# 56 expert blocks of two sizes in place of 55 of one size, with another order of products in the small ones

## What is computed

```python
X = np.fft.fft(np.fft.fft(x, axis=1), axis=2).real
# experts: D = 256, F = 1024, E = 8
expert_idx = np.argmax(logits, axis=1)
for e in range(E):
    mask = expert_idx == e
    h = np.maximum(x[mask] @ w1[e], 0.0)
    out[mask] = gate_w[mask, None] * (h @ w2[e])
# channel mix of 24 tiles of 512 tokens: x_k, x_r from x and the token before
k = np.maximum(xk @ w_k, 0.0)
v = k * k @ w_v
r = 1.0 / (1.0 + np.exp(-(xr @ w_r)))
return r * v
```

## Time and profile before

| | |
|---|---|
| median of three runs | 1440.82 us |
| profiled execution, its own time | 1442.9 us |
| its span, first to last instruction | 1440.9 us |
| busy: matmuls (PE) / VectorE (DVE) / ScalarE (ACT) / GpSimd (POOL) | 97% / 76% / 61% / 17% |
| mean granted TensorE clock | 0.989 |
| expert stage: products of the first and second layer, busy | 324.7 and 328.7 us |

### The profile page before, as it was taken

How to read it: one execution, slowest core, us unless ns; L and a number is a source line. 1 busy time by engine, 2 the same in 40 slices (tenths; PEclk the granted TensorE clock), 3 DMA queues, 4 the chain that set the end, 5 groups by cost and what they waited for, 6 DMA issues and landing times.

```text
span 1440.9 us, 27303 instructions
## 1 busy us (share of the span) xinstructions
PE 1403.9 (97%) x9048; PEld 1282.2 (89%) x9048; DVE 1088.1 (76%) x1815; ACT 872.3 (61%) x1687; POOL 250.8 (17%) x225
## 2 busy tenths in 40 slices
PE   8999989998999999999999969999999999999998
PEld 7988879998999999999999958888888888888886
DVE  4788887876776777777677657878788887878784
ACT  2665576665766666666666546656565666656563
POOL 2154537551331111111111100000000000000000
PEclk8999999999999999999999989999999999999999
DMA  8334378899667677777766322212131313131201
GB/s 243 84 102 130 119 240 277 270 292 322 221 212 226 218 219 218 228 240 235 227 216 219 132 45 40 49 32 55 29 58 29 58 29 58 29 58 29 57 17 29
DMA packets 208343, 201.49 MB, mean 140 GB/s; under 512 B 189641, under 2 KB 191543, under 8 KB 199672
## 3 DMA queue, kind: packets, MB, share of 16 engines
q1 hardware_dynamic: 197336, 175.18, 42.9%
q0 software_dynamic: 9888, 25.28, 5.3%
q10 hardware_dynamic: 1056, 0.26, 0.1%
HBM read 160.44 MB, written 42.06 MB: 141 GB/s over the span
## 4 chain that ended last, share of the span: by engine, by line
PE 91%; DVE 3%; DMA 2%; SPq 1%; ACT 1%; issue 1%; POOL 0%; ACTq 0%; POOLq 0%; DVEq 0%
PE ps L626 82%; PE ps L654 3%; PE ps L694 3%; PE ps L679 1%; DMA we_raw<-w_e 1%; PE ps L680 1%; DMA rows<-xr,pos 1%; DVE zu L1171 1%; DVE zv L1171 1%; SPq L455 0%; DVE we L1146 0%; SPq L540 0%; DMA xm<-moe 0%; ACT we L817 0%; PE ps L631 0%
## 5 line engine op out<-in xcount | busy, mean ns | idle before, releaser
L626 PE MATMUL ps<-x_split,w_split 128*128 128x512 f32 x1440 | 332.3, 391 | 11.3 <-DVE x_split L1293 11.3
L626 PE MATMUL ps<-we,ht 128*128 128x256 f32 x2640 | 328.7, 283 | 4.8 <-DVE ht L1229 4.8
L626 PEld LDWEIGHTS ps<-x_split,w_split 128*128 128x128 f32 x1440 | 271.6, 189 | 68.1 <-issue 11.5
L626 PE MATMUL ps<-xgt,we 128*128 128x256 f32 x2640 | 324.7, 282 | 4.3 <-DVE we L1146 4.3
L626 PEld LDWEIGHTS ps<-we,ht 128*128 128x128 f32 x2640 | 322.1, 189 | 6.4 <-DVE ht L1229 6.1
L626 PEld LDWEIGHTS ps<-xgt,we 128*128 128x128 f32 x2640 | 319.4, 190 | 4.7 <-issue 4.7
L1146 DVE TENSOR_TENSOR we<-we_raw,we 128x1024 fp32r<-128x1024 f32 x220 | 263.9, 1221 | 22.6 <-ACT we L817 22.1
L626 PE MATMUL ps<-k_split,w_split 128*128 128x512 f32 x1152 | 265.0, 389 | 0.0
L626 PEld LDWEIGHTS ps<-k_split,w_split 128*128 128x128 f32 x1152 | 216.2, 188 | 44.9
L1229 DVE SCALAR_TENSOR_TENSOR ht<-ps,ht 128x512 fp32r<-128x512 f32 x220 | 146.1, 684 | 144.4 <-ACT ht L878 144.2
L817 ACT CAST we<-we_raw 128x1024 fp32r<-128x1024 f32 x220 | 225.1, 1048 | 8.3 <-DMA we_raw<-w_e 8.3
(11 more groups left out here) (131 smaller groups left out, 1085.4 us busy)
## 6 DMA issues: line engine op xcount, KB each, us to landing
we_raw<-w_e SPq DMA_DIRECT2D x55, 2048.0 KB, 8.3
xg<-rows SPq DMA_DIRECT2D x220, 64.0 KB
out<-yc SPq DMA_DIRECT2D x96, 128.0 KB, 2.7
xm<-moe SPq DMA_DIRECT2D x94, 128.0 KB, 2.8
xin<-x SPq DMA_DIRECT2D x15, 768.0 KB, 6.5
rows<-tailc SPq DMA_DIRECT2D x9, 258.0 KB, 9.2
moe<-yo,meta POOLq DMA_INDIRECT x110
rows<-xr,pos POOLq DMA_INDIRECT x96, 2.7
```

The costliest lines, as they stand in the source:

```text
L626: ins = mm(o, a(i), b_(k), start=first_ and n == 0, stop=last_ and n == 2)
```

## The change

The constants now give 47 blocks of 256 tokens and 9 of 128 (`NS`), together `NB` = 56. `blocks` takes the place of `pairs`: 18 large blocks unrolled, then nine passes of a hardware loop with four blocks each (`MIX`), of which the fourth is small, then two large ones. The semaphore counts are rewritten with `at_`, `ahead`, `turn` and `scattered_ahead` for the two sizes; loads, transposes and scatters of a small block handle 128 tokens.

A small block's first layer uses each high weight once, with the high and the low part of the rows side by side as 256 columns, and each low weight with the 128 high columns. So a PSUM bank holds, for each of two slices, a half k=0 (high x high plus low x high) and a half k=1 (high x low). ScalarE copies the second half out (`half_b`), VectorE adds the first (`sum_one`), ScalarE makes the high part by a ReLU (`hidden_one`), VectorE the remainder (`low_one`). The second layer has one token half and 24 products.

The lists get a third kind of step. Large blocks of tier 2 are counted by rounding down, an expert with an odd half block gets one small block, and the small blocks left over are the halves of further large ones (`tier_odd`, `tier_odd2`, `tier_odd3`, `tier_spare`, `tier_spare2`, at the ends of VectorE's steps 7 to 11; `tier_a` to `tier_e` move to steps 4 to 6). The last of them adds the third count to `d_tier`, and `load_tails` waits for three. The diff, cut to its core:

```diff
-NB = B * S // BT + E - 1
-TIERS = ((0, 17), (17, 38))
+NS = 9
+NP = (B * S // P + E - 1 - NS) // 2
+NB = NP + NS
+MIX = 4
+TIERS = ((0, 17), (17, NP - 17))
+LIST = TIERS[1][1] + (NS + 1) // 2
...
+        def one(i):
+
+            return i[1] == MIX - 1 if isinstance(i, tuple) else LEAD <= i < LEAD + MIX * NS and (i - LEAD) % MIX == MIX - 1
+
+        def tokens(i):
+
+            return P if one(i) else BT
...
+        def blocks(eng, step):
+
+            for i in range(LEAD):
                 step(i, i % 2)
-            m = (n - lead - 1) // 2
-            with eng.Fori(0, m) as t:
-                for s in range(2):
-                    step(t * 2 + (lead + s), (lead + s) % 2)
-            for i in range(lead + 2 * m, n):
+            with eng.Fori(0, NS) as t:
+                for r in range(MIX):
+                    step((t, r), r % 2)
+            for i in range(LEAD + MIX * NS, NB):
                 step(i, i % 2)
 
...
             def load_meta(i, s):
 
-                r = sp.value_load(row_of[0:1, bass.ds(i, 1)], min_val=0, max_val=E * CAPR)
+                n = tokens(i)
+                r = sp.value_load(row_of[0:1, bass.ds(i, 1)], min_val=0, max_val=XROWS - n)
                 if i >= LEAD + 2:
-                    sp.wait_ge(scattered[s], i // 2 * (16 * HB))
-                sp.dma_start(meta_of(i, s)[:], rows[bass.ds(r, BT), D:ROW].rearrange("(j p) c -> p j c", j=HB)
+                    sp.wait_ge(scattered[s], scattered_ahead(i, s))
+                sp.dma_start(meta_of(i, s)[:, 0:n // P], rows[bass.ds(r, n), D:ROW].rearrange("(j p) c -> p j c", p=P)
                              ).then_inc(meta_in[s], 16)
...
             def load_tails():
 
-                sp.wait_ge(d_tier, 2)
+                sp.wait_ge(d_tier, 3)
...
+                n = tokens(i)
                 w1_ = [we[s][:, k, 0:DC * F].rearrange("p (c f) -> p c f", c=DC) for k in range(2)]
                 for f in range(FC):
                     if f % 2 == 0:
-                        wait(pe, m_hl, (i - 1) * (FC // 2) + (f // 2 + 1))
+                        wait(pe, m_hl, (at_(i) - 1) * (FC // 2) + (f // 2 + 1))
+                    if one(i):
+                        o = ps[:, f // 2, f % 2 * BT:(f % 2 + 1) * BT].rearrange("p (k t) -> p k t", k=2)
+                        for c in range(DC):
+                            hi, lo = [w1_[a][:, c, f * P:(f + 1) * P] for a in range(2)]
+                            if c == DC - 1:
+                                mm(o[:, 0, :], lo, xgt[:, 0, c, 0:P], start=False, stop=False)
+                            last = mm(o, hi, xgt[:, :, c, 0:P], start=(c == 0), stop=(c == DC - 1))
+                            if c < DC - 1:
+                                mm(o[:, 0, :], lo, xgt[:, 0, c, 0:P], start=False, stop=False)
+                        if f % 2:
+                            last.then_inc(m_up, 1)
+                        continue
                     for c in range(DC):
-                        last = mm3(ps[:, f // 2, (f % 2) * BT:(f % 2 + 1) * BT],
+                        last = mm3(ps[:, f // 2, (f % 2) * n:(f % 2 + 1) * n],
                                    lambda a: w1_[a][:, c, f * P:(f + 1) * P],
-                                   lambda k: xgt[:, k, c, :], c == 0, c == DC - 1)
+                                   lambda k: xgt[:, k, c, 0:n], c == 0, c == DC - 1)
...
+            def half_b(i, n):
+                act.wait_ge(m_up, at_(i) * (FC // 2) + (n + 1))
+                copy(h_b[n % 2], ps[:, n, :].rearrange("p (f k t) -> p f k t", f=2, k=2)[:, :, 1, :]).then_inc(m_hb, 1)
+
+            def hidden_one(i, n):
+                act.wait_ge(m_hs, i[0] * (FC // 2) + (n + 1))
+                if n == 0:
+                    wait(act, m_down, ahead(i, HB, 1))
+                nc.scalar.activation(ht[:, 0, 2 * n:2 * n + 2, 0:P], h_s[n % 3], ACT.Relu).then_inc(m_hh, 1)
+
+            def m_one(i, s):
+                half_b(i, 0)
+                w_high_part(after(i), 1 - s, 0)
+                half_b(i, 1)
+                hidden_one(i, 0)
+                half_b(i, 2)
+                hidden_one(i, 1)
+                w_high_part(after(i), 1 - s, 1)
+                half_b(i, 3)
+                hidden_one(i, 2)
+                hidden_one(i, 3)
+                rows_a(after(i))
+                w_high_part(after(i), 1 - s, 2)
+                w_high_part(after(i), 1 - s, 3)
+                result(i, s, 0)
...
+            def tier_spare2():
+
+                total_odd = sums[1][:, 4 + E:5 + E]
+                t_link(v.tensor_scalar(late1[:], iota[0:1, 0:NS], total_odd, None, ALU.is_ge))
+                for out_, h, none, dst in ((where1, 0, E * CAPR, row_of), (who1, 1, E - 1, expert_of)):
+                    t_link(v.scalar_tensor_tensor(out_[:], late1[:], -float(none), out_[:], ALU.mult, ALU.add))
+                    t_link(v.tensor_tensor(out_[:], out_[:], got1[:, h, :], ALU.add))
+                    end = copy(dst[:, mixed].rearrange("o (t r) -> o t r", r=MIX)[:, :, MIX - 1], out_[:])
+                end.then_inc(d_tier, 1)
...
+            def sum_one(i, n):
+                dve.wait_ge(m_hb, i[0] * (FC // 2) + (n + 1))
+                if n == 3:
+                    dve.wait_ge(m_hl, at_(i) * (FC // 2) + 1)
+                v.tensor_tensor(h_s[n % 3], ps[:, n, :].rearrange("p (f k t) -> p f k t", f=2, k=2)[:, :, 0, :], h_b[n % 2],
+                                ALU.add).then_inc(m_hs, 1)
+
+            def low_one(i, n):
+                h = [ht[:, k, 2 * n:2 * n + 2, 0:P] for k in range(2)]
+                dve.wait_ge(m_hh, at_(i) * (FC // 2) + (n + 1))
+                v.scalar_tensor_tensor(h[1], h_s[n % 3], 0.0, h[0].bitcast(F32), ALU.max, ALU.subtract).then_inc(m_hl, 1)
+
+            def m_one(i, s):
+                rows_t(after(i), 1 - s)
+                sum_one(i, 0)
+                sum_one(i, 1)
+                low_one(i, 0)
+                sum_one(i, 2)
+                low_one(i, 1)
+                w_low_part(after(i), 1 - s, 0)
+                sum_one(i, 3)
+                low_one(i, 2)
+                low_one(i, 3)
+                rows_v(after(i), 1 - s)
+                for q in range(1, WP):
+                    w_low_part(after(i), 1 - s, q)
...
                     if i == 4:
                         tier_a(True)
+                        tier_a2(True)
                     if i == 5:
-                        tier_a2(True)
+                        tier_b(True)
+                        tier_c(True)
                     if i == 6:
-                        tier_b(True)
+                        tier_d(True)
+                        tier_e(True)
                     if i == 7:
-                        tier_c(True)
+                        tier_odd()
                     if i == 8:
-                        tier_d(True)
+                        tier_odd2()
                     if i == 9:
-                        tier_e(True)
-
-            pairs(dve, LEAD, NB, m_step)
+                        tier_odd3()
+                    if i == 10:
+                        tier_spare()
+                    if i == 11:
+                        tier_spare2()
+
+            blocks(dve, m_step)
```

More of the change, by code:

```diff
@@ L256, in fft_moe_channel_mix @@
         assert at[0] <= cw_at
+        at[0] = 0
+        h_b = [part(f"h_b{n}", [2, P]) for n in range(2)]
+        h_s = [part(f"h_s{n}", [2, P]) for n in range(3)]
+        assert at[0] <= early
         at[0] = cw_at
@@ L742, in m_step @@
                 down(i, s)
-            pairs(pe, LEAD, NB, m_step)
+            blocks(pe, m_step)
             for n in range(2):
                 pe.wait_ge(s_split[n], len(C_SPLIT_AT))
-            pe.wait_ge(m_y, NB * HB)
+            pe.wait_ge(m_y, ahead(NB, HB, 1))
             def c_step(t, s):
@@ L890, in m_step @@
             def m_step(i, s):
+                if one(i):
+                    m_one(i, s)
+                    return
                 more = not isinstance(i, int) or i + 1 < NB
-                hidden_a(i, 0)
+                for n in range(FC // 2):
+                    hidden_a(i, n)
+                    if more and n < 2:
+                        w_high_part(after(i), 1 - s, n)
                 if more:
-                    w_high_part(i + 1, 1 - s, 0)
-                hidden_a(i, 1)
-                if more:
-                    w_high_part(i + 1, 1 - s, 1)
-                hidden_a(i, 2)
-                hidden_a(i, 3)
-                if more:
-                    rows_a(i + 1)
-                    w_high_part(i + 1, 1 - s, 2)
-                    w_high_part(i + 1, 1 - s, 3)
+                    rows_a(after(i))
+                    w_high_part(after(i), 1 - s, 2)
+                    w_high_part(after(i), 1 - s, 3)
                 if isinstance(i, int) and i in C_SPLIT_AT:
@@ L915, in m_step @@
                     exponential(B - 1)
-                for j in range(HB):
+                for j in range(tokens(i) // P):
                     result(i, s, j)
```

(45 more changed lines are left out.)

172 lines of the change are left out of this document (113 added, 59 removed).

## The result

The changed kernel takes 1464.66 us (median of 4 runs, 1462.04 to 1468.42) beside 1440.62 us for the kernel before (4 runs, 1439.21 to 1442.13): 1.0169 times as long, 95% interval 1.0144 to 1.0193. Forecast were 1470.6 us and a range of 1452 to 1486. The profiled execution of after took 1462.04 us (span 1460.1); that of before 1442.9 (span 1440.9). So the two traces differ by 19.2 us and the medians by 24.0: after's profiled execution is the shortest of its runs, and before's is longer than its other runs.

A forecast was written before the change was run, and what follows sets the result against it. TensorE, busy 97% of the span, was taken to bound the kernel. Loop +8.3 and lead +21.5 make 29.8 us: 1442.9 + 29.8 = 1472.7, from the 2.1 lower median 1470.6 us; range 1452 to 1486.

The forecast's parts named there:

- both mechanisms: Lead: tail stores on SP wait for the odd list, +21.5 us; loop: late weight loads hold up small blocks' followers, +8.3 us.
- Two large blocks in the loop: In the loop over experts, a large block takes 11.45 us, two take 22.9 us.
- The small block: In the loop, a small block takes 9.3 us, not the 6.5 us of TensorE alone.
- the timetable: Small block, engine by engine: TensorE done at 8.26 us, then waiting for VectorE's weight part 1 until 9.3.
- Its follower: Block behind a small one: its cast waits 2.1 us for weights landing at 13.6; the pair takes 22.55 us.
- The loop's sum: Loop after the lead: 9 x (22.55 + 22.9) + 22.9 = 432.0 us against 423.7, +8.3 us.
- The lead: First blocks: tails on SP wait for the odd list, delaying rows and weights queued behind; +21.5 us, bounds 14 to 24.
- The total: Whole kernel: 8.3 + 21.5 = 29.8 us more, 1470.6 us as median.
- The loads don't bind: Rival, loop: loads land sooner or ScalarE's order absorbs them; pair 20.75 us, loop -8 us, total 1454; chance 0.12.
- Faster: Rival, loop: small blocks cost only TensorE's 6.5 us; loop -33 us, total 1429 with the lead's loss; chance 0.05.
- The clock falls as well: Rival, loop: waits lower TensorE's clock, 1.5 us a fall; one each round +13 us, 1484, two 1497; chance 0.15.
- The cover of the lead: Rival, lead: its wait is covered, rows of 13 coming some other way; loop loss only, 1449; chance 0.06.

The follow-up runs named there:

- e7: e5 with the small blocks' first layer as 48 products of 128 columns, without halves; 1433.68 us, ratio 0.9861 to the kernel before.
- c1: The changed kernel run once more, unedited, on the chip of e9; 1467.71 us, ratio 1.0167 to the kernel before.
- e2: The changed kernel with the weight load of block i+2 issued ahead of block i+1's `meta` load, in the loop; 1444.11 us, ratio 1.0012.
- e4: The kernel before with the same reordering of loads as in e2; 1441.17 us, ratio 0.9989.
- c2: The kernel before run once more, unedited, on the chip of e9; 1445.97 us in its one run.
- e3: The kernel before with only a tiny VectorE copy ending step 11 as third signal, for which the tail stores wait; 1455.01 us, ratio 1.0089.
- e9: e5 with the first two weight parts of the block behind a small one made early; 1415.49 us, ratio 0.9806 to the kernel before.
- e5: The changed kernel with the edits of e1 and e2 together, on another chip; 1437.27 us, ratio 0.9888 to the kernel before.
- e8: e5 with only the first weight part of the block behind a small one made early; 1435.07 us, ratio 0.9861 to the kernel before.
- e1: The changed kernel with SP's eight tail stores moved from ahead of its iteration 11 to ahead of iteration 13; 1452.17 us, ratio 1.0070.

## Why the prediction was right

Time, direction and both mechanisms came out as forecast. The steps one by one:

- **Two large blocks in the loop.** 11.45 us before, 11.43 after; right.
- **The small block.** Forecast 9.3 us, measured 9.06. VectorE is last in it, as the timetable had it: TensorE waits 0.77 us for a remainder and 0.87 for the first weight part. The priced operations came out as 0.42 us (additions, remainders), 0.37 (copies) and 0.42 (ReLUs). A product of 128 columns, put at 0.11 between 0.06 and 0.119, is 0.1106 in e7. The row that this was taken from says less than it was read to say: 0.122 us for 96 columns is 2.7 times what its columns would make it (96/256 of 0.119), not twice, and its operands are plain float32, of which 290 columns take 0.245 us (0.98 us for four, 160.78 to 161.76 in after). That 0.11 fits so well is in part luck.
- **Its follower.** The pair was forecast at 22.55 us and takes 22.41 (c1: 23.19, three falls of the clock in it). The load goes out 4.79 us into the small block, not 5.4, and lands after 7.9 us rather than 8.2, so ScalarE waits 1.36 us in the block shown, not 2.1. e2 and e4 show that the load is the cause: moved ahead, it frees the follower and does nothing for the kernel before.
- **The loop's sum.** Forecast +8.3, measured +6.5: nine pairs at 0.14 less are 1.3 of the difference. In the second pair of traces (c1, c2) it is +13.4, with three falls of the clock in it.
- **The lead.** The chain is as forecast and e3 makes nearly all of it alone, but the sum is not: +21.5 forecast, +15.9 measured. In the first pair of traces this is the one mis-sized term. From the signal to the last tail it is 9.1 us rather than 11.0, since the tails go out on a queue that had been quiet: 8.14 us for the eight rather than 9.93. The prediction named that as its lower bound and took the row of before. The rows followed after 0.76 us rather than 1.4, weights 13 after 4.21 rather than 4.5, weights 14 after 12.32 rather than 12.7, and landed in 9.28 rather than 10.35. Together that is -4.2, and the cast moves by 17.3 us against block 10's start. The last 1.3 us: from that cast to block 14 it is 9.11 us rather than 10.45 in the earlier trace rows, since the fall of the clock of the earlier trace rows now came earlier, in block 12, where the next load hides it. The prediction carried it along as if it were fixed.
- **The total.** 8.3 + 21.5 = 29.8 forecast, 6.5 + 15.9 = 22.4 measured; the head's -4.2 and the rest's +1.0 make the 19.2 of the traces. The medians' 24.0 lie nearer to 22.4, and those of c1 and before on its chip differ by 25.6. So the forecast was 4 to 6 us too high. It was not further off because two errors have opposite signs: the lead was priced too dear, and falls of the clock in the loop, which come in some executions, were left out of the sum. That they offset is luck.
- **The rivals.** "The loads don't bind" would have needed followers of 11.45 us, and they take 13.35; that case is what e2 builds. "Faster" was tied to small blocks under 7.6 us with no loss behind them (7.8 by the prediction's own sum), the lead's loss still in it. Only e9 has such blocks, and it is faster, but so are e5, e7 and e8 with 8.2 to 8.6 us: all four lack the lead's loss, so this bound itself was not tested. "The clock falls as well" did not happen in after's trace, but it did in c1's, in 3 rounds of 9 at 1.7 to 2.0 us: the mechanism is real and its chance was too coarse a way to put it, since it belongs to the execution and not to the kernel. The Trainium skill, "TensorE: Matmul & The Clock Gate", section "HAM oscillation — how this bites in real kernels", tells of a loop in which every wait is longer than the products ahead of it, and in which every pass starts slow. The waits here are 0.2 to 1.5 us beside 11.4 us of products in a follower, so the prediction stretched that passage when it applied it to the small blocks; c1, with falls in 3 passes of 9, and after, with none, show that it does not hold here as it stands. The cover of the lead did not exist, as program order on SP said.

What stays open: on the chip of e5 to e8 the four traces show block 2 at 19.6 to 21.6 us rather than 13.1, and the kernel before is slower there by 13 us. The kernel before was not profiled on that chip, so the cause was not settled; comparisons there are to before's runs on that chip. What decides whether the clock falls in a given round is open too.

## What to carry to other kernels

Before you make blocks shorter, measure for each load how far it lands ahead of its use, and what its issue hangs on: a load that is just in time at one block length can take back what a shorter block saves, and here its repair was a change of order on the issuing queue, which cost nothing where it wasn't needed. A wait on a queue in program order delays all that is behind it, so put stores that nobody needs soon behind the loads that the next block needs, and look which load is then the next to be late. Here the order of products that saves work on TensorE paid only once the engines that feed those products were free of queued work in that moment; moving one of two queued parts away gave 2 to 4 us, moving both some 12.

## What the runs showed of the hardware

- The same eight stores, with the same register reads between them, take 8.14 to 8.25 us to issue where SP had been waiting for the signal (after, e2, e3, c1), and 9.89 to 10.41 where it had not (c2, e1, e5, e9). The price of an issue isn't a constant of the instruction; in the dear cases a weight load had been issued 1.1 to 1.6 us before the first store, in the others the queue had been quiet for 19 us or more, and which of the two counts was not separated.
- A product of 128 columns with its own weights costs 0.1106 us, one of 256 columns 0.119: halving the columns saves 7%.
- With nearly equal waits the clock falls in some executions and in some rounds, and not in others: in 3 of 9 followers in c1, in none in after; and within c1, behind waits of 0.72 and 0.76 us both times, at 660 us but not at 570. One trace without a fall can't rule it out.
- The head of the same kernel, up to block 12, took 330.29 us in one profiled execution and 333.57 in another, so a difference of 4 us between two traces can lie wholly ahead of the change.
